# A recurrence's triangular solve in blocks of 16 rows instead of 32, with one more level of joins on TensorE and another order of the work

## The reference, cut to what matters

```python
B, H, S, D = 4, 8, 768, 40
for t in range(S):
    y[:, :, t] = np.einsum('bhd,bhde->bhe', rt, state)
    Sa = np.einsum('bhde,bhe->bhd', state, at)
    state_decay = state * wt[:, :, None, :] - np.einsum('bhd,bhe->bhde', Sa, bt)
    state = state_decay + np.einsum('bhd,bhe->bhde', vt, kt)
# then, twice, with N = 3072 tokens, E = 8 experts, D = 320, F = 1024:
e_idx = np.argmax(x @ w_gate, axis=1)
out[token] = gate_w[token] * (np.maximum(x[token] @ w1[e], 0) @ w2[e])   # e = e_idx[token]
# (the first layer has an output gate, the second a capacity per expert)
```

## Time and profile before

| | us |
|---|---|
| median of 3 runs | 1383.2 (1378.79 to 1397.67) |
| profiled execution | 1393.2 |
| its span, first to last instruction | 1391.1 |
| mean granted clock of TensorE, share of full | 0.823 |
| busy: PE / PEld / DVE / ACT / POOL | 1034.3 / 877.2 / 699.4 / 259.5 / 401.9 |
| recurrence, until the first instruction of L1025 | 590.5 |

### The profile page before, as it was taken

How to read it: one execution, slowest core, us unless ns; L and a number is a source line. 1 busy time by engine, 2 the same in 40 slices (tenths; PEclk the granted TensorE clock), 3 DMA queues, 4 the chain that set the end, 5 groups by cost and what they waited for, 6 DMA issues and landing times.

```text
span 1391.1 us, 39572 instructions
## 1 busy us (share of the span) xinstructions
PE 1034.3 (74%) x16688; PEld 877.2 (63%) x16689; DVE 699.4 (50%) x1261; ACT 259.5 (19%) x476; POOL 401.9 (29%) x350
## 2 busy tenths in 40 slices
PE   1446677566775776780699999998622999997996
PEld 1445677566675666640588888887302888886884
DVE  5699999889998876133123223232140332322331
ACT  0222343334332343220011011010100101100010
POOL 4333523545243521105222212222024122211211
PEclk8567776767766677685799999999765999999998
DMA  2626444555545332042133333330502223344000
GB/s 79 153 69 155 112 116 122 128 134 136 118 115 135 84 72 49 4 151 81 58 106 111 100 109 112 101 113 28 175 30 96 77 68 108 111 125 153 33 28 0
DMA packets 166574, 134.02 MB, mean 96 GB/s; under 512 B 102442, under 2 KB 143918, under 8 KB 164912
## 3 DMA queue, kind: packets, MB, share of 16 engines
q1 hardware_dynamic: 147088, 102.18, 27.5%
q10 hardware_dynamic: 12096, 14.09, 3.4%
q0 software_dynamic: 7264, 15.86, 3.1%
HBM read 99.79 MB, written 34.58 MB: 97 GB/s over the span
## 4 chain that ended last, share of the span: by engine, by line
PE 58%; DVE 15%; DMA 9%; issue 7%; SPq 4%; POOL 2%; ACT 2%; POOLq 0%; ACTq 0%; DVEq 0%
PE pair L1092 18%; PE pair L1073 16%; DVE products L1164 7%; PE pair L1080 5%; DVE T_rows L1169 4%; PE pair L1035 2%; DMA t_dram<-T_rows 2%; PE pair L1060 2%; PE bank L958 2%; POOL x_sorted L590 2%; DMA g_dram<-G_b 2%; PE bank L965 2%; DMA abk_in<-w 1%; DMA G_rows<-g_dram 1%; PE pair L1025 1%
## 5 line engine op out<-in xcount | busy, mean ns | idle before, releaser
L1092 PE MATMUL pair<-abk_in,G_rows 128*128 x992 | 278.5, 434 | 1.7 <-DVE y_T L1340 1.7
L1073 PEld LDWEIGHTS pair<-y_T,rvm 128*128 128x128 f32 x1984 | 238.5, 197 | 21.0 <-issue 8.5
L1073 PE MATMUL pair<-y_T,rvm 128*128 128x128 f32 x1984 | 239.8, 281 | 9.9 <-DVE rvm L1325 7.6
L1092 PEld LDWEIGHTS pair<-abk_in,G_rows 128*128 128x128 f32 x992 | 183.6, 190 | 72.0 <-issue 2.7
L1164 DVE TENSOR_TENSOR products<-T_rows,G_rows 128x4 f32<-128x4 f32 (+30 forms) x372 | 213.8, 575 | 12.4
L540 POOL TENSOR_SCALAR_AFFINE_SELECT rvm<-rvm 64x1024 f32<-64x1024 f32 x48 | 76.4, 1591 | 272.1 <-ACT rvm L631 270.5
L1325 DVE COPY rvm<-AG 128x2560 f32 x62 | 95.3, 1537 | 100.7 <-issue 73.9
L1169 DVE TENSOR_REDUCE T_rows<-products 128x2 f32<-128x4 f32 (+30 forms) x372 | 133.8, 360 | 12.8
L757 ACT ACTIVATE G_rows<-pair 128x512 f32<-128x512 f32 x62 | 37.0, 597 | 527.8 <-PE pair L1080 527.8
L1332 DVE TENSOR_SCALAR G_rows<-pair 128x512 f32<-128x512 f32 x62 | 42.7, 689 | 148.8 <-PE pair L1080 148.8
L1060 PE MATMUL pair<-table_sb,y_T 128*128 128x128 f32 x186 | 34.5, 295 | 92.2 <-DMA y_T<-x_sorted 92.2
(11 more groups left out here) (135 smaller groups left out, 1463.3 us busy)
## 6 DMA issues: line engine op xcount, KB each, us to landing
abk_in<-w SPq DMA_DIRECT2D x16, 1280.0 KB
G_rows<-g_dram SPq DMA_DIRECT2D x48, 256.0 KB
y_T<-x_sorted ACTq DMA_DIRECT2D x62, 160.0 KB, 2.2
AG<-w SPq DMA_DIRECT2D x16, 512.0 KB
AG<-w SPq DMA_DIRECT2D x32, 256.0 KB
x_sorted<-empty SPq DMA_DIRECT2D x6, 1288.0 KB, 6.3
AG<-w SPq DMA_DIRECT2D x32, 128.0 KB
w_in<-wT SPq DMA_DIRECT2D x48, 80.0 KB
```

The lines of the kernel that those rows point to most:

```text
L1073: mm(to, w1_now[:, par, k * F + m * P:k * F + m * P + P], xT[:, (0, 2 - m // 4)[k], :], start=(m % 4 == 0 and k == 0), stop=False, skip_gr ...
L1092: last = mm(bank[5][:, 0:DM], hidT[par][:, k, :], ring2[:, bass.ds(place, 1), k, :].rearrange("p a d -> p (a d)"), start=(k == 0), stop=(k ...
```

## The change

The solve works on diagonal blocks of 16 x 16. The 32 matrices of a set, with two sides (the heads' place in a PSUM pair) and four blocks each, are 128 systems of 16 rows, one on each partition, with nothing held twice. Rows t = 1 to 15 are solved, and T is also kept in natural order (T_nat). A new pair of joins on TensorE makes blocks of 32 out of blocks of 16: `join_first` multiplies, `ga_out` copies to A_sb, `join_second` multiplies by D_nat, and `t16_out` copies into T_T in four pieces. `quotient` and `corner` then join to 64 as before.

The transfers: `send_g` has eight DMAs instead of four, `fetch_g` one instead of four, `send_t` two instead of four, `fetch_t` twelve (eight to T_T, four to D_nat) instead of four.

The order: `quotient` of a set moves from the chain's first half to the end of the slot before; `grams_k` and its eviction of the second half go behind `state`; on VectorE the first eight rows open the slot, and the last seven stand behind y_out and state_out of the first half; `turn_first` waits for the new copies and stands ahead of the second state_out. On SP the T transfers move ahead of the loads of r, v, a, b and k, and b and k now also wait for gk_ready. The expert layers' tile hidT moves from the space of G_rows to that of H_nat. The diff, cut:

```diff
-EARLY_ROWS, FIRST_ROWS = 9, 22
-ROWS_STEPS = 2 * HALF
+BLK = 16
+NBLK = C // BLK
+SOLVE_STEPS = 2 * (BLK - 1) + 1
+T_DMAS = 3 * NBLK
+FIRST_ROWS = 9
...
+            blocks = [(h, n) for n in range(NBLK) for h in range(2)]
...
             def send_g(k):
-                for blk, h in quarters:
+                for h, n in blocks:
...
             def fetch_g(k):
-                for n in range(4):
-                    sp.dma_start(G_rows[n * 32:(n + 1) * 32, k % 2].rearrange("p h t j -> p (h t j)"),
-                                 g_dram[k % 2].rearrange("b x h t j -> (b x) (h t j)")).then_inc(g_landed, 16)
+                sp.dma_start(G_rows[:, k % 2].rearrange("p t j -> p (t j)"),
+                             g_dram[k % 2].rearrange("h n x t j -> (h n x) (t j)")).then_inc(g_landed, 16)
 
             def send_t(k):
...
+                sp.dma_start(t_dram[k % 2].rearrange("h n x s t -> (h n x) (s t)"),
+                             T_rows[:, k % 2].rearrange("p s t -> p (s t)")).then_inc(t_sent, 16)
+                sp.dma_start(tn_dram[k % 2].rearrange("h n x t s -> (h n x) (t s)"),
+                             T_nat[:, k % 2].rearrange("p t s -> p (t s)")).then_inc(t_sent, 16)
 
             def fetch_t(k):
                 u = 2 * k % 4
-                for blk, h in quarters:
+                for h, n in blocks:
+                    pair_at, data_at = n // 2 * HALF, (1 - n % 2) * BLK
                     sp.dma_start(
-                        T_T[rows_of(blk, h), u:u + CC, :, :, blk * HALF:(blk + 1) * HALF].rearrange(
+                        T_T[rows_of(h, n), u:u + CC, :, :, pair_at:pair_at + HALF].rearrange(
                             "q c o a t -> q (c o a) t"),
-                        t_dram[k % 2, blk, :, h].rearrange("x s q t -> (s q) x t")
+                        t_dram[k % 2, h, n, :, :, data_at:data_at + HALF].rearrange("x s t -> s x t")
                         ).then_inc(t_landed[k % 2], 16)
+                for h, n in blocks:
+                    if n % 2 == 0:
+                        sp.dma_start(D_nat[rows_of(h, n), :, :],
+                                     tn_dram[k % 2, h, n].rearrange("x t s -> t x s")
+                                     ).then_inc(t_landed[k % 2], 16)
...
+            def join_first(k):
+                pe.wait_ge(t_landed[k % 2], 16 * T_DMAS * (k // 2 + 1))
+                if k + 1 < NK:
+                    pe.wait_ge(gb_copied, k + 2)
+                pe.wait_ge(gk_copied, 2 * (2 * k + 1))
+                for m in range(2):
+                    for c in range(CC):
+                        for a in range(NPAIR):
+                            for o in range(2):
+                                for h in range(2):
+                                    at = (c * H + o * NPAIR + a) * BLK
+                                    q = SIDE[h] + m * HALF
+                                    last = mm(pair[1][q:q + BLK, h, at:at + BLK],
+                                              G_b[q:q + HALF, k % 2, c, o, a, m * HALF:m * HALF + BLK],
+                                              T_T[q:q + HALF, (2 * k + c) % 4, o, a, m * HALF + BLK:(m + 1) * HALF],
+                                              start=True, stop=True)
+                last.then_inc(ga_ready, 1)
+
+            def join_second(k):
+                pe.wait_ge(ga_copied, 2 * (k + 1))
+                pe.wait_ge(nat_copied, 2 * k + 2)
...
             for j in SLOTS:
-                solves, starts, loads = live_sets(j + 1, j + 2, j + 3)
...
+                solves, loads = live_sets(j + 1, j + 3)
+                chain = 0 <= j < NK
+                if solves:
+                    solve_first(j + 1)
+                if 0 < j <= NK:
+                    y_out(2 * j - 1)
+                if chain and has_next(2 * j):
+                    state_out(2 * j)
+                if solves:
+                    solve_last(j + 1)
                 if loads:
                     decays(j + 3)
...
+                if chain:
+                    y_out(2 * j)
                 if solves:
                     turn_first(j + 1)
+                if chain and has_next(2 * j + 1):
+                    state_out(2 * j + 1)
```

More of the change, by code:

```diff
@@ L98, in tables @@
     row = np.arange(P)
-    for s in range(8):
-        t["solve_init"][row, s * HALF + s * 4 + row // 32] = 1
+    t["solve_init"][:, ::BLK + 1] = 1
     t["earlier"] = (j < i).astype(np.float32)
@@ L990, in _ @@
                         right_side(u)
-                        state_natural(u)
-                    if nats:
-                        grams_k(u + CC)
-                        natural(u + CC)
-                    if chain and c == 0:
-                        quotient(j)
-                    if 0 <= u - 1 < NU:
-                        outputs(u - 1)
-                    if chain and c == 0:
+                    if c == 0 and chain:
                         corner(j)
@@ L1003, in _ @@
                     if chain:
+                        state_natural(u)
+                    if c == 0:
+                        if nats:
+                            grams_k(u + CC)
+                        if 0 <= u - 1 < NU:
+                            outputs(u - 1)
+                        if nats:
+                            natural(u + CC)
+                    else:
+                        if nats:
+                            natural(u + CC)
+                        if 0 <= u - 1 < NU:
+                            outputs(u - 1)
+                        if nats:
+                            join_first(j + 1)
+                    if chain:
                         solved(u)
@@ L1006, in _ @@
                             state(u)
+                    if c == 1 and nats:
+                        grams_k(u + CC)
+                        join_second(j + 1)
+                    if chain:
                         inner(u)
+                    if c == 1 and nats:
+                        quotient(j + 1)
                     if c == 0 and 0 < j <= NK:
```

202 lines of the change are left out of this document (119 added, 83 removed).

## The result

The changed kernel takes 1464.6 us (median of 4 runs, 1461.65 to 1467.65) against 1382.3 for the kernel before (4 runs, 1378.79 to 1397.67). The recorded ratio is 1.057, 95% interval 1.050 to 1.064 (the medians alone give 1.060): slower. The forecast of 1430 us had the direction and the mechanism, and the time lies within its wide range (1372 to 1470), but it was 35 us short, and the time lies above the 1410 to 1460 that it gave as its own.

A forecast was written before the change was run, and what follows sets the result against it. VectorE, full before, would give way to a serial loop of 12.0 + 17.7 + 18.5 = 48.2 us a slot; the recurrence, 73.9 + 524.6 + 38.3 = 636.8 against 590.5, gave 1430 us, range 1372 to 1470.

The forecast's parts named there:

- its own list: Signs expected in the new profile, such as VectorE near 22 us a slot, plus findings that would prove it wrong.
- costed at nothing: send_g and fetch_g, 8.4 us, taken as covered by the wait for outputs; up to 5 if uncovered.
- first E: First time the first-level join is back in T_T (each such moment is called E): forecast at 73.9 us.
- eleven slots: Recurrence after the first E: 48.2 us each, 530.2, less 3.6 outputs and 2.0 scaling absent at the ends: 524.6 us.
- tail: Recurrence's end after the last slot: old 33.3 us plus 5.0 for inner, right side and state-in-natural: 38.3.
- A, landed to E: From T's landing in T_T to the joins' results copied back there: joins, solved, state, grams_k, copies; 12.0 us.
- B, E to st_ready: TensorE's chain from the joins' results in T_T, inner through state, until state_out is released: 17.7 us.
- collisions with GpSimd: Last seven solve rows on VectorE, slowed by GpSimd's masks and scaling: taken as 1.5 us a slot.
- the slowest rival: 1.2 GHz in state too, joins at 30 ns, a product caught twice: slot 55.2 us, 1506 us; chance 0.11.
- the last line of the sum: Carried the profiled run's 10 us over the median across, giving 1430 us from the recurrence's +46.
- The rival "faster": TensorE held at 2.4 GHz from the landing on, its idle share shrinking: slot 40.6 us, 1346 us; chance 0.11.
- the bounds from the rows: Each join on TensorE, estimated from 32-column passes in the earlier trace: 1.1 to 3.8 us, taken 2.2.

The follow-up runs named there:

- rows_first: Changed kernel with the solve's last seven rows and T_nat copy ahead of the slot's first y_out and state_out: 1417.4 us, 1.021 of before.
- filled_wait: Changed kernel with nine matmuls of constants filling TensorE's wait for T in each slot: 1470.2 us, 1.060 of before.
- g_early: rows_first with SP's send_g and fetch_g right behind fetch_t, ahead of the loads of r, v, a, b and k: 1386.7 us, 1.003 of before.
- joins_twice: Changed kernel with every product of join_first and join_second issued twice, in place: 1561.8 us, 1.129 of before.
- g_merged: g_early with join_second as one product of 48 rows instead of two of 16, zeros in D_nat off the diagonal: 1372.1 us, 0.992 of before.
- g_swap: g_merged, with two of four join-result copies moved to VectorE, then join_second and its copies put ahead of grams_k: 1355.2 us, 0.979 of before.

## Why the prediction was right, and where its size was off

**Mechanism.** Right, by most of its own list. VectorE's work per slot is 24 us (forecast near 22); TensorE stands 7.7 to 11.4 us before join_first, ended by D_nat (8 to 11); the T_T and D_nat issues spread over 5.7 us (4.5 to 6); the last seven rows start 0.03 us behind state_out; the joins took 1.8 and 1.7 us (taken 2.2, and "wrong" only over 3 or under 1.5). G's transfers, costed at nothing, stayed off the loop in the slot shown: VectorE waits 5.6 us for them, and still stands 2.33 us before state_out. rows_first shows by removal that the place behind state_out was the main cost. Two entries of the list failed. From quotient to quotient it said 46 to 50 us, and the eight full slots take 50.9 (from join_first to join_first). And it called itself wrong if the clock was up before outputs, which it was, for a short stretch (see the clock below).

**The sum.** Measured against forecast, in the recurrence: first E 77.2 (73.9), eleven slots 552.1 (524.6), tail 33.8 (38.3). The error of 26 us is in the slots. Means of eight full ones:

| stretch | forecast | measured | mis-sized term |
|---|---|---|---|
| A, landed to E | 12.0 | 12.8 | stops for instructions, 1.5 (at most 2.5); joins 0.9 cheaper |
| B, E to st_ready | 17.7 | 18.6 | the same stops, 0.8 (at most 1.6) |
| state_out to T_nat's end, over the 6.3 for state_out and rows | 1.5 | 2.6 | collisions with GpSimd, now on three products |
| send_t | 3.6 | 3.3 | |
| fetch_t | 7.1 | 7.2 | |
| slot | 48.2 | 50.9 | |

The stops were known from one row (1.52, in the earlier trace rows) and I subtracted them where I read durations, so that each price was that of a group which never stops. In a loop in series those in A and B are on the path, 2.3 us a slot and some 26 us of the 41 over the recurrence; the rest fall beside the last rows and the transfers and cost nothing. I put them only into the slowest rival. The collision was bounded at 0 to 2.3, taken at 1.5 and is 2.6, for both kinds come in every full slot: the scaling catches the product of 196 elements (1.53 over the 0.36 of its reduction, priced 1.3) and the masks those of 144 and 169 (0.81 and 0.86 us beside a 0.30 and a 0.33 reduction, 1.0 in all, priced at up to 1).

**The level.** 13 us more came from the last line of the sum: I took the profiled run's 10 us over its median as lasting, but the profiled run of after lies 3 us under its own median. With 26 from the recurrence, less 4 behind it, that is the 35. It was not luck that the direction held, for the place behind state_out alone is worth 47 us; but in the slot only the joins and the send were priced too dear and all else too cheap, and the time stayed inside 1470 only because that bound was set by the slowest rival.

**The clock.** Right in level for most of A and for B (granted 0.50 to 0.52 from 415.6 to 424.8, 0.50 from 428.1 to 440.2) and wrong in detail: from 424.8 to 428.1, join_second and the copies, it was 0.99 in the slot shown, and six of the eight full slots have such a stretch at 1.00 inside A. The rival "faster" rested on less standing before the joins; filled_wait removed that standing, and the time did not fall.

**The rule that was set aside.** The prediction cites the Trainium skill (TensorE: Matmul & The Clock Gate, "Wait — 56ns, not 53.3ns?") for at least 25 ns from start to start. Within a burst the trace does not agree: it stays at 13 to 14 ns for 16 columns, at 1.2 GHz (1.82 us for 128) and at 2.4 (g_early, 370.4 to 371.3, clock 1.00, 63 passes in 0.90 us). In the changed kernel the joins cost 1.8 and 1.7 us, between the bounds from the rows (1.1 to 3.8), and not the 3.2 of that rule. Here products that follow each other use different rows of the array (`h` is the innermost loop); whether that is the reason is not shown. Only in joins_twice, with 256 passes in a row, do the stops bring the mean to 23 ns.

## What to carry to other kernels

When an engine that is full is relieved by a step that starts at another engine's end, add up the loop, transfers included, before counting what each engine saves; here VectorE saved 190 us and the kernel lost 82. Where matmuls are tiny, count instructions as well as busy time: a merged product with zeros in it and as much busy time went with a faster kernel. Once the loop is cut, look again at which wait ends last: the last three gains (1.1, 0.5 and 0.7%) came with fewer stops for instructions and then, in two steps, with a shorter wait for the copies.

## What was not expected of the hardware

- TensorE ran out of instructions in dense runs of thin passes: +50 us of stops for 3072 more passes, one packet of 16384 bytes for 128 passes of 14 ns, 1.8 us of work. In both traces every stop ended 1.2 to 1.6 us behind the end of such a packet.
- A pass of 16 columns takes 12 to 15 ns from start to start at either clock; a join_first of 128 passes took 1.75 us to the next start at 1.2 GHz (changed kernel, 415.61) and 1.62 at 2.4 (filled_wait, 419.38).
- A product of 48 rows and 48 columns of weights takes about as long as two of 16 at 2.4 GHz and longer at 1.2 (768 passes in 23.9 us in g_merged and 29.8 in g_swap, against 22.5 for 1536).
- Large matmuls in a wait lifted the granted clock to 1.00 there and behind it, and the next busy stretch of thin ones still fell to 0.56.
